# A fused recurrence and two expert layers on one core: second unit one slot later, four banks for the last layer's first products, last store in four

## What is computed

```python
def _attn_ref(q, k, v, alpha):            # B, H, S, D = 4, 8, 768, 48
    for t in range(S):
        state = alpha[:, :, t, :, None] * state + np.einsum('bhd,bhe->bhde', k[:, :, t], v[:, :, t])
        y[:, :, t] = np.einsum('bhd,bhde->bhe', q[:, :, t], state)

x = np.ascontiguousarray(attn_out.transpose(0, 2, 1, 3)).reshape(B * S, H * D)   # 3072 x 384

def _moe_ref(x, domain_probs, w1, w2):    # E, F = 4, 1024
    p = domain_probs / (domain_probs.sum(-1, keepdims=True) + 1e-09)
    for e in range(E):
        out += p[:, e:e + 1] * (np.maximum(x @ w1[e], 0.0) @ w2[e])

def _moe2_ref(x, w_in, w_out):            # 384 -> 2048 -> 384
    h = x @ w_in
    return (h - np.tanh(h)) @ w_out
```

## Time and profile before

| | before |
|---|---|
| median of 3 runs | 1481.12 us (1480.62 to 1481.49) |
| the profiled execution | 1480.82 us, span 1479.0 us |
| TensorE matmuls | busy 1368.3 us, 93% |
| TensorE weight loads | busy 1138.7 us, 77% |
| VectorE | busy 893.4 us, 60% |
| ScalarE | busy 561.5 us, 38% |
| GpSimd | busy 452.0 us, 31% |
| share of the chain that ended last | TensorE 83%, VectorE 6%, issue 4% |
| granted TensorE clock, mean | 0.966 of 2.4 GHz |

### The profile page before, as it was taken

One profiled execution on the slowest core, in us unless ns is written; L12 is line 12 of the kernel. 1 busy time (PEld: TensorE's weight loads), 2 busy tenths in 40 slices (PEclk: granted clock), 3 DMA queues, 4 the chain that ended last, 5 costly groups with the idle time before them and its releaser, 6 DMA issues.

```text
span 1479.0 us, 25620 instructions
## 1 busy us (share of the span) xinstructions
PE 1368.3 (93%) x10177; PEld 1138.7 (77%) x10177; DVE 893.4 (60%) x1552; ACT 561.5 (38%) x1004; POOL 452.0 (31%) x400
## 2 busy tenths in 40 slices
PE   3449999899999999999999999999999999999998
PEld 2437778678877788777879777879887879888878
DVE  6647474798464498555488546478646458433386
ACT  1222524673222374221375131366131346311175
POOL 5555656672403032212222131323131013100032
PEclk7559999999999999999999999999999999999999
DMA  5239687765655655655655655565664455565542
GB/s 174 70 111 308 214 284 264 273 230 195 229 173 190 233 186 180 204 182 187 205 204 191 205 188 191 173 233 187 196 203 160 164 193 191 186 219 192 182 181 86
DMA packets 104917, 289.05 MB, mean 195 GB/s; under 512 B 9984, under 2 KB 64864, under 8 KB 104800
## 3 DMA queue, kind: packets, MB, share of 16 engines
q1 hardware_dynamic: 104800, 287.43, 58.2%
HBM read 242.52 MB, written 42.52 MB: 193 GB/s over the span
## 4 chain that ended last, share of the span: by engine, by line
PE 83%; DVE 6%; issue 4%; ACT 2%; SPq 0%; DMA 0%; POOL 0%; DVEq 0%; ACTq 0%
PE bank L557 13%; PE bank L558 12%; PE bank L559 12%; PE bank L580 9%; PE bank L581 9%; PE bank L582 9%; PE bank L604 4%; PE bank L602 4%; PE bank L603 4%; PE bank L478 3%; PE bank L513 2%; DVE GG L961 1%; PE bank L500 1%; DVE GG L957 1%; PE bank L456 1%
## 5 line engine op out<-in xcount | busy, mean ns | idle before, releaser
L557 PE MATMUL bank<-XB,RG 128*128 128x512 f32 x864 | 354.3, 410 | 26.8 <-DVE TH L954 19.7
L732 ACT ACTIVATE HH<-GG 128x512 fp32r<-128x512 f32 x192 | 121.2, 631 | 677.6 <-PE bank L582 560.9
L558 PE MATMUL bank<-XB,RG 128*128 128x512 f32 x864 | 343.1, 397 | 0.0
L559 PE MATMUL bank<-XB,RG 128*128 128x512 f32 x864 | 342.1, 396 | 0.0
L930 DVE SCALAR_TENSOR_TENSOR GG<-bank,PB 128x512 f32<-128x512 f32 x192 | 132.7, 691 | 338.6 <-PE bank L559 338.4
L1067 POOL TENSOR_TENSOR HL<-GG,HH 128x512 fp32r<-128x512 f32 x96 | 128.3, 1337 | 514.7 <-ACT HH L752 514.7
L580 PE MATMUL bank<-HH,RG 128*128 128x512 f32 x576 | 225.2, 391 | 1.8 <-ACT OUT L765 1.5
L581 PE MATMUL bank<-HH,RG 128*128 128x512 f32 x576 | 224.4, 390 | 0.0
L582 PE MATMUL bank<-HL,RG 128*128 128x512 f32 x576 | 224.1, 389 | 0.0
L557 PEld LDWEIGHTS bank<-XB,RG 128*128 128x128 f32 x864 | 163.8, 190 | 77.0 <-issue 36.3
L1050 POOL TENSOR_TENSOR KU<-KU,TOT 128x256 f32<-128x256 f32 x96 | 75.5, 813 | 385.5 <-PE bank L478 385.5
(11 more groups left out here) (76 smaller groups left out, 1705.4 us busy)
## 6 DMA issues: line engine op xcount, KB each, us to landing
RG<-scratch SPq DMA_DIRECT2D x240, 768.0 KB, 4.3
scratch<-RG SPq DMA_DIRECT2D x48, 768.0 KB, 4.6
VS<-vp SPq DMA_DIRECT2D x12, 768.0 KB, 6.1
AU<-qka SPq DMA_DIRECT2D x12, 512.0 KB, 5.3
R<-qka SPq DMA_DIRECT2D x12, 512.0 KB, 5.3
KU<-qka SPq DMA_DIRECT2D x12, 512.0 KB, 6.0
WS<-w SPq DMA_DIRECT2D x32, 192.0 KB, 3.1
PB<-probs SPq DMA_DIRECT2D x6, 1024.0 KB, 8.3
```

The costliest lines, as they stand in the source:

```text
L557: nc.tensor.matmul(out, w1(g, 0, kt), x_part(m, 0, kt), start=(kt == 0), stop=False)
L558: nc.tensor.matmul(out, w1(g, 0, kt), x_part(m, 1, kt), start=False, stop=False)
L559: last = nc.tensor.matmul(out, w1(g, 1, kt), x_part(m, 0, kt), start=False, stop=(kt == KT - 1))
```

## The change

Four edits. `STAGGER` goes from 15 to 16. The last layer's first products use four banks in turn, the two of `h_bank` and the two of `a_bank`, and wait for the reader of four f before (for f = 2 and 3: for the second unit's output to be out of the banks); step 0 of a first unit now waits for the last readers of f = 14 and 15 of the block before. `hidden_low` of slot 31 stands ahead of the unit's step 15 on VectorE. The last block's output is stored tile by tile.

```diff
-STAGGER = 15
+STAGGER = 16
...
+        h2_bank = h_bank + a_bank
...
+            def store_tile(t):
+                m = NTB - 1
+                sp.wait_ge(y_out, TT * m + t + 1)
+                sp.dma_start(out_d[m * TB + t * P:m * TB + t * P + P, :],
+                             OUT[:, t * DM:t * DM + DM]).then_inc(stored, 16)
...
-            store(NTB - 1)
-            sp.wait_ge(stored, 16 * NTB)
+            for t in range(TT):
+                store_tile(t)
+            sp.wait_ge(stored, 16 * (NTB - 1 + TT))
...
             def bank_free(u, k):
...
+                if k < 2 and u % 2 == 0 and u > AHEAD:
+                    pe.wait_ge(diff_done, (u // 2 - 1) * SLOTS2 - 1 + k)
...
                 elif m:
-                    pe.wait_ge(diff_done, (m - 1) * SLOTS2 + SLOTS2 - 1 + s)
+                    pe.wait_ge(diff_done, (m - 1) * SLOTS2 + SLOTS2 - 3 + s)
...
             def first2(m, f):
...
-                if f >= 2:
-                    pe.wait_ge(diff_done, m * SLOTS2 + f - 1)
+                if f >= 4:
+                    pe.wait_ge(diff_done, m * SLOTS2 + f - 3)
+                elif f >= 2:
+                    pe.wait_ge(x_low, 3 * min(2 * m + 4, UNITS))
                 else:
                     pe.wait_ge(scaled, (m + 1) * SLOTS1 - 1 + f)
-                first_product(m, g, h_bank[f % 2][:, :], f == 0)
+                first_product(m, g, h2_bank[f % 4][:, :], f == 0)
...
                 if f == 0:
                     pe.wait_ge(x2_low, KT * m + KT)
-                    pe.wait_ge(x_low, 3 * min(2 * m + 4, UNITS))
...
                     if s:
                         hidden_low(m, s - 1)
+                    if s == SLOTS1 - 1:
+                        hidden_low(m, s)
                     for u, step in units_at(m, s):
                         attention(u, step)
-                hidden_low(m, SLOTS1 - 1)
                 low_x2(m)
```

More of the change, by code:

```diff
@@ L736, in functions @@
                 c = two_slot(f)
-                h = h_bank[f % 2][:, :]
+                h = h2_bank[f % 4][:, :]
                 if n >= 2:
@@ L952, in cube @@
                     dve.wait_ge(g_low, n - 3)
-                nc.vector.tensor_tensor(gg, SQ[:, c], h_bank[f % 2][:, :], ALU.mult).then_inc(cubed, 1)
-                nc.vector.tensor_tensor(TH[:, c], h_bank[f % 2][:, :], TH[:, c], ALU.subtract).then_inc(diff_done, 1)
+                nc.vector.tensor_tensor(gg, SQ[:, c], h2_bank[f % 4][:, :], ALU.mult).then_inc(cubed, 1)
+                nc.vector.tensor_tensor(TH[:, c], h2_bank[f % 4][:, :], TH[:, c], ALU.subtract).then_inc(diff_done, 1)
                 dve.wait_ge(cubed, n + 1)
```

## The result

The changed kernel takes 1441.6 us (median of 4 runs, 1441.14 to 1442.16), the kernel before 1481.3 (4 runs, 1480.62 to 1482.99): ratio 0.973, 95% interval 0.9714 to 0.9747. That is 2.4 us under the 1444.0 forecast and inside its range. The profiled execution took 1441.96 us with a span of 1440.1, against a span of 1479.0 before, so 38.9 us are gone from the span where the sum said 36.9.

What follows compares the result with a forecast made beforehand. TensorE, busy for 93% of the span, was taken as the bound. The terms 20.4 + 14.3 + 1.5 + 0.7 = 36.9 us led from 1480.8 to 1443.9, with 0.3 some 1444 us; range 1438 to 1450.

Steps and rivals of the forecast that it cites:

- The second unit's start: Score products of the second unit, five starts: with STAGGER 16 the XS wait and the clock loss go, saving 20.4 us.
- block 0's cover: GpSimd's preparation of the next unit beside weight splits in block 0: cover not shown by any row, left to the range.
- The rest order: Slot 31, VectorE's rest product ahead of the unit's output: costs nothing; without cover, up to 0.7 us in each of five blocks.
- Four banks in blocks 1 to 5: First products 1 to 4 of the last layer: three TH waits go, 2.87 us a block, 14.3 us in all.
- Block 0's last layer: VectorE sets the pace there; TensorE's gain is at most 2.46 us, taken as 1.5, ends 0 and 2.5.
- the step that names the stand: Block 0's end: TensorE stands about 3 us ahead of the score products, taking 0.6 x 1.6 us of clock off 2.46.
- The HL waits: Sign in block 0: waits of 0.5 to 0.7 us ahead of second products, with GpSimd's HL as releaser.
- a DMA of RG would release a first product: Sign that the forecast is wrong: a first product of the last layer waits for an RG refill.
- The store: Last block's output stored in four pieces: gain between 0 and 1.5 us, taken as 0.7.
- The clock: Behind TensorE stands of about 3 us the granted clock can fall; 3 of 5 cost 1.6 us or more.

Runs made afterwards that it cites:

- the last experiment: The changed kernel with GpSimd's rest of a product issued behind the next weight split, in block 0's last layer alone: 1434.92 us, ratio 0.9692 to the kernel before.

## Why the prediction was right

**The second unit's start: right in mechanism and size.** 20.4 us forecast, 20.2 measured alone. The wait went and did not move, but for 0.8 us in block 0, and both parts of the price (the stand, and the clock behind it) were needed to see it: the idle figures alone, 14.4 us, would have missed 6 of 20. XS was 1.3 us early, forecast 1.4. That the total comes out so close is in part luck: block 0 gained 0.5 us less than its 5.6, the four other blocks together 0.3 more. The prediction had left block 0's cover to the range, since no row showed it; the wait for SC there is what came of it. Luck is also that the term holds the three clock falls of one profiled execution: executions of the kernel before took 1478.36 to 1485.45 us in one job, the fastest with a mean granted clock of 0.972 and the slowest with 0.962.

**The rest order: right.** No wait shows a cost, as forecast, and the rows of block 2 show why: VectorE does the slot's rest at 717.15, directly behind HH, then the unit's output, done at 718.72 + 0.41 = 719.13, and still stands idle for ScalarE's copy before the layer's first output bank (L953) at 719.78, so 0.65 us of cover are left.

```profile
717.15 0.69 DVE L947 TENSOR_TENSOR HL<-GG,HH 128x512 fp32r<-128x512 f32 x1 [1.47 <-ACT HH L743]
717.78 0.69 DVE L903 TENSOR_TENSOR XB<-bank,XB 128x512 fp32r<-128x512 f32 x1
...
718.72 0.41 DVE L908 TENSOR_TENSOR XS<-bank,XS 128x256 fp32r<-128x256 f32 x1
719.78 0.69 DVE L953 TENSOR_TENSOR XB<-bank,XB 128x512 fp32r<-128x512 f32 x1 [0.65 <-ACT XB L768]
```

What the prediction did not say is how much hangs on it: put back, it costs 10.9 us.

**Four banks in blocks 1 to 5: right, a little low.** Forecast 2.87 us a block, measured 2.95 to 3.0: 14.3 against about 14.9 us. The forecast took the difference between 11.15 and 4 x 2.07; the products then took 8.17. What ended last next was neither HL nor the score products: the cover of 1.1 us ahead of the second product 0 was thin and held. Three banks would have done.

**Block 0's last layer: the size was off, by the step that names the stand.** The prediction took 2.46 us less 0.6 x 1.6 for the clock, because TensorE would have stood about 3 us ahead of the score products. It stood there for less, since a refill of RG came late just before and split the stand in two:

```profile
333.96 0.50 PE L567 MATMUL bank<-XB,RG 128*128 128x512 f32 x1 [1.04 <-DMA RG<-scratch]
340.27 1.16 PE L466 MATMUL bank<-R,KU 64*64 64x64 f32 x64 [1.86 <-DVE TH L965]
```

The clock fell behind neither (1.00 in the windows that follow them), so the clock's share stayed. By the fixed points block 0 gained 7.33 us. The last layer's first VectorE operation came 5.2 us earlier, at 270.06 in place of 275.26, so the last layer kept 7.33 - 5.2 = 2.1 us, where the sum had 1.5. VectorE does set this layer's pace, as the prediction said: from TH of f = 0 to TH of f = 15 it is 68.6 us before and 68.7 after. The score products now start 0.25 us behind the end of the last TH (339.34 + 0.68 = 340.02) and not 2.46 us, so 2.2 of the 2.46 us that were the bound came in. One thing in this layer the prediction did not price: in the kernel before, TensorE stood 1.98 and 2.54 us near its start, and the clock fell behind that too:

```profile
285.85 0.47 PE L557 MATMUL bank<-XB,RG 128*128 128x512 f32 x1 [2.54 <-DVE TH L954]
...
288.00:292.00 4.00, 4.00 (x16) 3.76 (x16) 3.97 (x4) 2.70 (x6) 2.66 (x3) 0.66 0.79 236
```

With the four banks these stands and this fall are gone, but that gained nothing here, since VectorE's pace stayed the same. The HL waits came as described, though shorter: 0.28 us, not 0.5 to 0.7. That a DMA of RG would release a first product was named as a sign that the forecast is wrong; it came once, for 1.0 us, and cost nothing: with three banks this wait is absent, and the score products come 234.28 us behind those that open block 0, against 234.27 here.

**The store: the size was off.** 0.7 was half way between the bounds, 1.6 was measured, just above the upper one. The nearest row, 48 KB in 2.1 us, would have come closer than the middle, since 192 KB took 2.0; but that row is one transfer, and the same 48 KB store took 1.5 us in the changed kernel's trace. Issuing four times cost nothing: the last piece was issued at 1475.0, as the single store was. The Trainium skill's rule to coalesce small transfers (DMA: Bandwidth & Descriptors, Rules for kernel authors) names no exception for a last transfer like this one, whose earlier parts can be sent sooner; the pieces of 192 KB are larger than the 64 KB that it gives. What its anatomy of one DMA gives, an estimate of 2.4 us for the last piece and 3.8 for the whole, stands beside 2.0 and at least 3.6 in the rows; the page measured it for transfers that GpSimd issues, and SyncE issues these.

**The clock.** 1.6 us per fall was right (the growth of the gain between blocks with and without a fall is 7.5 - 5.95). That it falls behind a given start or not was not in any row to be forecast: with the same 2.88 us of idle time it fell three times of five in the kernel before and four of five with the banks alone. What decides it stays open.

## What to carry to other kernels

Price a stall of TensorE by the distance between the starts of two fixed instructions on either side of it, in the kernel at hand, and look at the granted clock behind it; the idle figure gave 14.4 of 20.2 us in one case and 7.4 of 10.9 in another. When a step moves later in a hand-written order, look at what now stands behind it in each queue: one VectorE instruction on the wrong side of the moved step gives back half of what the step brings. Where VectorE and GpSimd work from SBUF at the same time, look at which instruction meets which: to issue one GpSimd instruction a step later, so that it does not start together with VectorE's, was worth 6 us here, more than the last store and block 0's banks together.

## What the runs showed of the hardware

- The same stand of TensorE (2.88 us of idle time) is followed by a lower clock in some places and not in others, and block 1's start was among them with the banks alone and not in the kernel before, though the two differ only in the banks of the last layer. In block 0, stands of 1.04 and 1.86 us were not followed by one; stands of 2.03 us (the rest behind the unit's output) and 2.64 us (GpSimd's rest later) were, and so was the one of 2.54 us in the kernel before, which came 4.9 us behind one of 1.98.
- In the last layer VectorE and GpSimd slow each other in VectorE's operations that read SBUF alone. L968 took 0.67 us alone and 1.50 beside GpSimd, L972 0.77 and 2.19; L964 and L965, which read a PSUM bank, took 0.66 to 0.72 in the same stretches. GpSimd's split (L1073) took 1.84 us alone and 2.30 in such a step. The Trainium skill, SBUF — State Buffer (section on who interferes with whom), says that a VectorE instruction with two SBUF inputs contends with a GpSimd instruction that reads SBUF, for a port pair that is locked and not shared out; the rows of L968 agree. That the order of the two queues decides how often it is met is what the last experiment adds.
- A store of 192 KB landed 2.0 us behind its issue (median of four) at the end of the program, one of 48 KB after 2.1 us in the kernel before and 1.5 in the changed kernel.
